# Key values of both streams in one slot; weighted values and state products of both in another slot, which stands between the two up products of its step

## What is computed

```python
for t in range(S):                        # r, k, v, w: (B, H, S, D) = (4, 8, 768, 48)
    cur = einsum('bhd,bhe->bhde', u[None] * kt, vt)
    y[:, :, t] = einsum('bhd,bhde->bhe', rt, state + cur)
    state = wt[:, :, :, None] * state + einsum('bhd,bhe->bhde', kt, vt)
x = y.transpose(0, 2, 1, 3).reshape(B * S, H * D)    # 3072 x 384
x = ((x @ w_a) * (x @ w_b)) @ w_out                  # gated layer, width 1536
h = x @ w_in                                         # leaky layer, width 2048
out = (maximum(h, 0) + alpha * minimum(h, 0)) @ w_out2
```

## Time and profile before

| | us |
|---|---|
| median of 3 runs | 1019.99 (1018.7 to 1020.4) |
| profiled execution, its own time | 1017.5 |
| profiled execution, its span | 1015.7 |
| TensorE matmuls busy in the span | 994.5 (98%) |
| VectorE busy | 559.8 (55%) |
| ScalarE busy | 288.6 (28%) |
| granted TensorE clock, mean over the span | 0.998 of full speed |

### The profile page before, as it was taken

How to read it: one execution, slowest core, us unless ns; L and a number is a source line. 1 busy time by engine, 2 the same in 40 slices (tenths; PEclk the granted TensorE clock), 3 DMA queues, 4 the chain that set the end, 5 groups by cost and what they waited for, 6 DMA issues and landing times.

```text
span 1015.7 us, 27744 instructions
## 1 busy us (share of the span) xinstructions
PE 994.5 (98%) x11776; PEld 971.7 (96%) x11776; DVE 559.8 (55%) x1170; ACT 288.6 (28%) x604; POOL 24.4 (2%) x24
## 2 busy tenths in 40 slices
PE   5899999999999999999999999999999999999998
PEld 5799999999999999999999999999999999999998
DVE  7686655655656646556432437555545454555554
ACT  3435314223242241331222334222121222222212
POOL 4500000000000000000000000000000000000000
PEclk9999999999999999999999999999999999999999
DMA  6644401312113013110020413010101010101000
GB/s 162 167 135 120 117 14 35 109 30 64 53 29 92 25 31 91 52 38 2 26 60 1 138 35 125 1 47 1 47 1 47 1 46 0 46 4 43 15 11 24
DMA packets 42130, 52.96 MB, mean 52 GB/s; under 512 B 5152, under 2 KB 42016, under 8 KB 42016
## 3 DMA queue, kind: packets, MB, share of 16 engines
q1 hardware_dynamic: 40624, 51.04, 17.3%
q10 hardware_dynamic: 1392, 0.25, 0.2%
HBM read 39.48 MB, written 9.44 MB: 48 GB/s over the span
## 4 chain that ended last, share of the span: by engine, by line
PE 96%; DVE 1%; issue 1%; ACT 0%; ACTq 0%; DMA 0%; SPq 0%; DVEq 0%
PE products L166 18%; PE products L167 16%; PE products L168 16%; PE acc L168 12%; PE acc L166 12%; PE acc L167 12%; PE products L694 5%; PE products L736 1%; PE products L752 1%; PE products L671 1%; PE products L708 1%; PE products L721 1%; DMA x_parts<-f_y 0%; DVE k_in L927 0%; DVE a_sb L944 0%
## 5 line engine op out<-in xcount | busy, mean ns | idle before, releaser
L166 PE MATMUL products<-x_parts,weights_hi 128*128 128x384 f32 x576 | 200.9, 349 | 4.1 <-DMA x_parts<-f_y 1.9
L167 PE MATMUL products<-x_parts,weights_hi 128*128 128x384 f32 x576 | 194.2, 337 | 0.0
L168 PE MATMUL products<-x_parts,weights_lo 128*128 128x384 f32 x576 | 193.9, 337 | 0.0
L1235 DVE TENSOR_SCALAR leaky_low<-products,leaky_al 128x384 f32<-128x384 f32 x128 | 79.0, 617 | 169.4 <-PE products L168 169.3
L1095 DVE TENSOR_TENSOR g_sb<-a_g,products 128x384 f32<-128x384 f32 x96 | 53.2, 554 | 191.4 <-issue 129.5
L1182 ACT ACTIVATE leaky_g_hi<-leaky_g_sb 128x384 fp32r<-128x384 f32 x128 | 67.2, 525 | 295.0 <-DVE leaky_g_sb L1240 295.0
L514 ACT ACTIVATE g_hi<-g_sb 128x384 fp32r<-128x384 f32 x96 | 50.3, 524 | 254.1 <-DVE g_sb L1095 254.1
L166 PEld LDWEIGHTS products<-x_parts,weights_hi 128*128 128x128 f32 x576 | 108.1, 188 | 8.9 <-issue 5.3
L167 PEld LDWEIGHTS products<-x_parts,weights_hi 128*128 128x128 f32 x576 | 108.2, 188 | 0.0
L168 PEld LDWEIGHTS products<-x_parts,weights_lo 128*128 128x128 f32 x576 | 108.2, 188 | 0.0
L168 PE MATMUL acc<-g_hi,weights_lo 128*128 128x384 f32 x288 | 97.5, 338 | 0.0
(11 more groups left out here) (85 smaller groups left out, 1747.7 us busy)
## 6 DMA issues: line engine op xcount, KB each, us to landing
k_in<-in_k_dram SPq DMA_DIRECT2D x16, 336.0 KB, 3.9
r_in<-in_r_dram SPq DMA_DIRECT2D x16, 336.0 KB, 4.8
stage<-in_w_out_dram SPq DMA_DIRECT2D x14, 384.0 KB, 3.1
w_v<-in_v_dram SPq DMA_DIRECT2D x16, 288.0 KB, 3.5
y_dram<-x_in SPq DMA_DIRECT2D x8, 576.0 KB, 3.0
x_in<-y_dram SPq DMA_DIRECT2D x8, 576.0 KB, 4.4
out_dram<-leaky_out_sb SPq DMA_DIRECT2D x7, 576.0 KB, 3.3
stage<-in_w_dram SPq DMA_DIRECT2D x10, 336.0 KB, 3.8
```

The source lines that it names most:

```text
L166: pe.matmul(out, w_hi, x_hi, start=first, stop=False)
L167: pe.matmul(out, w_hi, x_lo, start=False, stop=False)
L168: return pe.matmul(out, w_lo, x_hi, start=False, stop=last)
L1235: dve.tensor_scalar(self.low[f % 2][:, :], h, 0.0, self.al[:, f:f + 1], ALU.min, ALU.mult).then_inc(self.low_ready, 1)
```

## The change

For duos 1 to 7 the key values of both streams go into the slot of phase 8, phase 9 has no slot, and phase 10 does the weighted values of both streams and the state products. The phase 10 slot (`lone_slot`) moves: it comes after `up_a` and before `up_b` of its step, and the `down` of the step before comes after `up_b`, as behind every step without a slot. VectorE carries the states of both streams in phase 8. In phase 9 the `w_b` result goes to bank 0 or 1, where the key values of stream 0 were, so that `up_b` waits for `states_done[0]`. In phase 10 it goes to bank 4. Duo 0 is as it was.

```diff
 def slot_at(g):
-    return g >= 0 and step_at(g) is not None and step_at(g) % PHASES != 1
+    return g >= 0 and step_at(g) is not None and step_at(g) % PHASES not in (1, 9)
+
+def lone_slot(g):
+    return slot_at(g) and step_at(g) % PHASES == 10
 
 def shared_bank(g):
-    return slot_at(g - 1) and slot_at(g)
+    return slot_at(g) and (slot_at(g - 1) or lone_slot(g))
...
                     else:
+                        weighted_values(n, 0)
                         weighted_values(n, 1)
...
                     elif phase == 8:
                         key_values(n, 0)
-                    elif phase == 9:
+                        if n > 0:
+                            key_values(n, 1)
+                    elif step == 9:
                         key_values(n, 1)
                         weighted_values(n, 0)
...
+                    elif step_at(g) % PHASES == 9:
+                        pe.wait_ge(states_done[0], states_after(step_at(g) // PHASES))
                     elif not shared_bank(g):
...
+                    if lone_slot(g):
+                        pe.wait_ge(g_ready, g)
+                        attend(step_at(g))
                     if slot_at(g - 1):
                         down(g - 1)
                     if g > 0:
                         up_b(g)
                     if g > 0 and not slot_at(g - 1):
                         down(g - 1)
-                    if slot_at(g):
+                    if slot_at(g) and not lone_slot(g):
                         pe.wait_ge(g_ready, g)
                         attend(step_at(g))
...
                     elif phase == 8:
                         carry_states(n, 0)
+                        if n > 0:
+                            carry_states(n, 1)
                     elif phase == 9:
-                        carry_states(n, 1)
+                        if n == 0:
+                            carry_states(n, 1)
```

## The result

The changed kernel takes 1021.12 us (median of 22 runs, 1017.3 to 1023.39) against 1018.53 for the kernel before (22 runs, 1016.39 to 1020.59). The ratio is 1.0024, 95% interval 1.0016 to 1.0031. It is slower by 2.6 us, where faster was forecast, and the time lies outside the range. The forecast of 1016.8 was counted from a median of three runs, 1019.99; from 1018.53 the same gain would give 1015.3. The profiled execution of the changed kernel took 1019.3 us, with a span of 1017.5; the one before had 1017.5 and 1015.7.

A forecast was written before the change was run, and what follows sets the result against it. TensorE was taken as the bound, busy 994.5 of 1015.7 us. Savings of 1.23 us (three even duos) and 1.96 (four odd) sum to 3.2, taking 1019.99 to 1016.8; range 1014.8 to 1019.6.

The forecast's parts named there:

- The turns: TensorE going between big and small products: one slot fewer a duo saves 0.10 + 0.09 + 0.10 = 0.29 us.
- the upper bound: Total saving if the two key-value groups abut more closely, up to 0.08 us more a duo: 3.8 us.
- The rule of free turns: Rival, chance 0.07: weight loads pulled ahead make turns free, so only phase 8's wait is saved, 1.2 us, time 1018.8.
- The hidden wait in phase 8: Unlisted wait of `up_a` for `g_ready` behind phase 8's slot; joining covers it: 0.12 us per even duo, 0.20 odd.
- The new waits: Waits for states, phase 9's multiplication and outputs: forecast to cost nothing, slacks 0.44, 0.7 (0.35 in duo 1), 0.5 us.
- Instruction supply: Rival, chance 0.05: slots of 2.8 us each meet a hole of 0.64, 4.5 us in all, time 1021.3.
- The sum: Slots of phases 8 to 10 counted before and after: 0.41 us less per even duo, 0.49 per odd, 3.2 in all.
- late states: Rival, chance 0.06: stream 0's states come late for phase 9's `up_b`, 0.75 us of waiting a duo, about 1022.5.

The follow-up runs named there:

- experiment 6: Kernel before with key values of both streams joined in phase 8's slot, phase 9 keeping a slot for weighted values: 1017.10 us, ratio 0.9984.
- experiment 3: Changed kernel with 22 tiny matmuls (88 instructions) put ahead of the first leaf: 1020.17 us, ratio 1.0014 to the kernel before.
- experiment 8: Kernel before with 24 tiny matmuls added in phase 10's slot of duos 1 to 7, no work moved: 1029.69 us, one run.
- experiment 2: Kernel before with the change made in duos 2, 3, 6 and 7 alone: 1021.57 us, ratio 1.0036.

## Why the prediction was wrong

**The turns.** Right in kind, and too small in even duos. I gave a duo 0.41 or 0.49 us. Hole-free duos of the changed kernel gained 0.45 (duo 1), 0.61 (duo 4) and 0.52 (duo 5). The term that was mis-sized is the slot of phase 8 in an even duo: 1.39 was forecast and 1.23 measured, because two groups of key values abut; in an odd duo it is 1.21 for 1.23. Three even duos at 0.61 and four odd ones at 0.49 would be 3.8 us, the upper bound. The rule of free turns, with 1.2 us in all, is refuted: experiment 6 keeps the turns, and in duos 1, 4 and 5 the change has 0.25, 0.35 and 0.37 us more than it, where 0.29 was forecast for a turn.

**The hidden wait in phase 8.** Right in all: 1.2 us forecast, 1.5 measured in experiment 6. The split is not as forecast. Even duos gained 0.17 to 0.29 us for 0.12, since the abutting groups come on top there, and odd ones 0.15 to 0.20 for 0.20, since 0.05 of the wait stays in phase 9.

**The new waits.** Right: in the changed kernel's list of waits TensorE waits for states once, in duo 0, and for the multiplication once, as before, and for no output.

**Instruction supply.** This is the step that failed. The sum has no term for holes. The prediction put them into a rival with a chance of 0.05 and gave as the reason that "slots of 2.09 and 2.16 have none". I took holes for accidents that strike a slot now and then, with 0.64 us of idle time at most, and argued from shorter slots. Measured were phase 10 slots of 4.17, 4.07 and 4.60 us in duos 2, 3 and 7, where 2.78 and 2.85 are enough, and 0.6 us behind that of duo 6. That is 5 us of holes against 3.8 us of savings, and each hole of the first three eats the saving of two or three duos.

What decides is the next fetch. TensorE passes a boundary at the earliest 2.36 us after the fetch's start, and in these duos that start came 0.58 to 1.12 us behind the boundary before, while the slot used up 256 rows in 2.0 us. A slot of 288 rows holds a whole block in an eighth of all positions, one of 352 or 384 in three eighths or half. So the length of the slot sets how often a block is used up so fast, and the start of the fetch whether that makes a hole. The row of the trace on which I based the rival was itself at such a boundary, and counting rows up to it would have led there.

That the rival's 1021.3 is so near to the measured 1021.12 is luck. It had seven holes of 0.64 us, and the trace has four, larger ones and a lowered clock. Another figure among the rivals does not add up: seven times 0.75 us less 3.2 is 2.0, so late states would give 1022.0, not 1022.5.

**The clock.** Not in the prediction at all. A hole with 1.49 us of idle time was followed by 3 us at the lower clock in duo 7. The same came after the hole of 1.51 in duo 1 of experiment 3 and after that of only 0.47 in duo 4 of experiment 8. It did not come after those of about 1 us in duos 2 and 3 of the changed kernel (the view of windows gives 1.00 from 160 to 175 and from 230 to 245), nor after that of 1.75 in duo 7 of experiment 2. So the length of a hole does not tell whether the clock falls. How much of the 2.6 us between the two medians comes from it in the runs without a trace stays open; the runs' mean clocks say that drops beyond the usual one are frequent (14 of 22).

Also open is why some fetches begin ahead of the boundary before and others up to 1.1 us behind it, and why the delay of the one for row 4801 varies, and with it the gap there: a start 3.9 us behind the boundary left a gap of 0.04, one 5.4 us behind it a gap of 1.50.

## What to carry to other kernels

Before small matmuls are gathered into one stretch, count their instructions, four for an f32 matmul with its weights here, and compare them with a block of 256: the slots of phases 8 to 10 with at most 288 rows had no hole in duos 1 to 7 of any trace, those with 352 to 384 had gaps of 0.5 to 2.0 us, or none, by where the boundary fell and how early the next fetch began. Gather up to that length, and put a block of big products in between when it is exceeded. A shorter stretch is not safe next to large loads: the slots of 192 rows in phase 3 of duo 2 had gaps up to 1.50. A gap without a semaphore is worth a count of the instructions up to it; several gaps at one place modulo 256 name their cause.

## What the runs showed that was not expected

A change far away, 88 or 172 instructions at the start, moved holes from duos 2, 3, 6 and 7 to duos 1, 5 and 6, or to 3, 4 and 5. So the place of the holes depends on the number of instructions ahead. The times were 1.0024, 1.0014 and 1.0007 of the kernel before for the same work and order, with intervals that overlap. From the start of a fetch's transfer to the next instruction it took 2.7 us in duo 2, while no other transfer was under way.
